# A fused attention, gated-MLP and convolution kernel: one tile of the output projection, parts of the first batch's softmax, and the second MLP's weight prefetch are put at other places in their engines' orders

## The chip, the cores and the metric

One NeuronCore of a Trainium2 chip runs the whole program. The metric is the device time of one execution in microseconds (us), the median over several executions; lower is better. The program has five instruction streams that run side by side and meet only at semaphores: TensorE (PE, matrix products; its weight loads are listed as PEld), VectorE (DVE), ScalarE (ACT), GpSimd (POOL) and SyncE (SP, which here only issues DMAs). ACT issues some DMAs too.

## The reference

```python
# q, k, v: (8, 8, 576, 64); first MLP: w_in 512x1024, w_out 512x512, w_sg 576x576;
# second MLP: w_in2 512x1024, conv_w 3x1024, w_out2 1024x512
q_s = exp(q - max(q, -1)); q_s = q_s / (sum(q_s, -1) + 1e-9)      # softmax over the head's 64
k_s = exp(k - max(k, 2));  k_s = k_s / (sum(k_s, 2) + 1e-9)       # softmax over the sequence
kv = einsum('bhsd,bhse->bhde', k_s, v)
x = einsum('bhsd,bhde->bhse', q_s, kv)           # then heads side by side: (8, 576, 512)
h = gelu_tanh(x @ w_in); u, v = h[..., :512], h[..., 512:]
v_n = (v - mean(v)) / sqrt(var(v) + 1e-6) * g_ln
v_s = einsum('ts,bsd->btd', w_sg, v_n) + b_sg[None, :, None]
x = x + (u * v_s) @ w_out
h = maximum(x @ w_in2, 0)
conv_out = sum over k of conv_w[k] * h shifted by k - 1 along the sequence
out = (h * sigmoid(conv_out)) @ w_out2
```

## The kernel before

The kernel goes through the eight batches of the first MLP (with the attention in front of it) one after another, and then through the eight batches of the second MLP. Each of its float32 matrix products is made of three passes over operands that are split in two parts: a "hi" part that ACT writes by rounding (functions named `hi_...`) and a "lo" part, the difference, that DVE writes (functions `lo_...`). A matrix product of 128x128 by 576 columns is thus three passes of two matmuls with 288 columns each, six matmuls of line L549.

In the first part, `body(m, a, n)` of each engine works on batch m, on the attention of batch a = m + 1, and on the first softmax steps of batch n = m + 2. Batch 0 has a `first_attention()` and its own branches (`start`); batch 7 has `a is None`. Nothing schedules this at run time: every engine's order is the order in which its function is written, and each step waits for semaphores (`e.wait_ge`) that other engines' steps raise. A wait blocks everything behind it on its engine.

The steps that matter here, for batch m and with f from 0 to 3 for four tiles of 128 gated features:

- PE: `sg_unit(m, f)` makes the sequence mixing of tile f (its last matmuls are line L715). Then `o_part(m, d, fs)` adds the products of the gated tiles `fs` to output block d, six matmuls for each f. Before its first tile f it waits for `g_lo` of that tile, `o_part(m, 1, ...)` first waits for `sg_affine` of tile 3 (line L1526) and `o_part(m, 2, ...)` for `kv_lo` (line L1450) of the next batch. After that come `x_piece(a, 0)` and the last output block. In batch 0 the PE also transposes the next batch's q (`turn_q`, L610, which needs `q_norm`, and from the third on `q_lo`) and multiplies exp(k) by v (`kv_piece`, L628, which needs `k_exp`).
- DVE: `affine(m, f)` (L1526) reads the result of `sg_unit`, `lo_g(m, f)` (L1533) writes the lo part of a gated tile and raises `g_lo`, `lo_q_rows(a, d)` (L1430) writes a lo part of the next batch's q, `add_x(m, d)` (L1550 and L1557, for the last block L1542 and L1547) adds the residual and raises `o_add` and `o_last`, and `lo_w2(n)` (L1571) writes a lo part of the second MLP's weights. In batch 0, `sum_q` (L1342, L1345, L1348) makes the reciprocal of a softmax sum, and `lo_w_out` is L1515.
- POOL: `gate(m, f)` (L1882) multiplies the tile by the affine result. In batch 0, `sub_q` (L1821) and `sub_k` (L1839) subtract the maxima of two tiles or the last one, and `scale_q` (L1826) multiplies by the reciprocal.
- ACT: exponentials, hi parts, `gelu`, and `store_x1(m, d)` (L1016), which issues the DMA that stores output block d of the first MLP from one of two buffers `x1`. `add_x(m, 2)` and `add_x(m, 3)` wait for the landing of the stores 0 and 1 of the same batch before they write those buffers again. `hi_w2(n)` (L1021) writes a hi part of the second MLP's weights.
- SP: after the last load for the attention it loads the eight chunks of the second MLP's weights (L518) through three staging buffers, with the first x of the second MLP (`load_x2(0)`, 1152 KB, L505) and the move of batch 7's tail (`move_tail`, L449) between them. Before the first chunk it waits for all `q_lo`, and then for this:

```python
            for x in x1_out:
                e.wait_ge(x, 32 * (B - 2) + 16)
```

With B = 8 this is met when stores 0 and 1 of batch 6 have landed. Chunks 3 and later each wait for `w2_lo`, which `lo_w2` raises.

## Time and profile before

| | us |
|---|---|
| median of 3 executions | 910.94 |
| lowest, highest | 910.55, 912.44 |
| profiled execution, its own time | 912.44 |
| profiled execution, span from first to last instruction | 910.6 |
| PE busy | 894.2 (98%) |
| DVE, ACT, POOL busy | 620.2, 398.4, 368.7 |

The profiled execution is one of the three: its own time is 1.8 us over its span, and 1.5 us over the median. The first MLP with the attention takes the span up to about 503 us, batch 0 up to about 94 us and each of the batches 1 to 6 some 59.4 us; the rest is the second MLP. The page lists work by line and engine; the timeline lists instructions with their start, their duration, and in brackets how long the engine was idle before them and who ended that. Durations in it include time in which an instruction stood still after it had started.

### The profile page before, as it was taken

The numbers are of one execution on the slowest core, as the hardware profiler recorded it, in microseconds if no ns is written. First come the engines' busy times: TensorE is split into PE (matmuls) and PEld (weight loads), VectorE is DVE, ScalarE is ACT, GpSimd is POOL, SyncE is SP. The second block draws the span as 40 slices with busy tenths as digits, with TensorE's granted clock in tenths as the row PEclk, the third lists the DMA queues.
The fourth block names the chain that finished last, engine by engine and source line by source line (L and its number), as shares of the span: only waits on it lengthen the run. The fifth ranks groups of instructions, "written<-read, shape, count | busy, mean of one in ns | idle before, by whom it ended". The sixth has DMA issues, their size and how long they took to land.

```text
span 910.6 us, 15155 instructions
## 1 busy us (share of the span) xinstructions
PE 894.2 (98%) x6132; PEld 831.8 (91%) x6132; DVE 620.2 (68%) x952; ACT 398.4 (44%) x593; POOL 368.7 (40%) x233
## 2 busy tenths in 40 slices
PE   6999999999999999999999999999999999999998
PEld 5798899999999999999999999999999999998986
DVE  6787958578597585875656797866575676757550
ACT  6652553445445445355254354434343343434331
POOL 5764566354572753736232133232232222232220
PEclk9999999999999999999999999999999999999999
DMA  9726674565554735553232202110202020200001
GB/s 298 217 85 203 197 203 147 146 189 171 157 197 127 216 120 154 165 157 83 95 131 70 106 1 87 55 44 12 87 13 87 24 76 24 76 24 24 24 34 47
DMA packets 60037, 99.59 MB, mean 109 GB/s; under 512 B 6720, under 2 KB 25408, under 8 KB 58304
## 3 DMA queue, kind: packets, MB, share of 16 engines
q1 hardware_dynamic: 55360, 89.20, 32.0%
q10 hardware_dynamic: 4608, 9.44, 2.7%
q8 instruction: 48, 0.79, 0.4%
q14 instruction: 21, 0.17, 0.1%
HBM read 78.46 MB, written 19.11 MB: 107 GB/s over the span
## 4 chain that ended last, share of the span: by engine, by line
PE 91%; DVE 3%; POOL 2%; issue 2%; ACT 1%; DMA 1%; SPq 0%; POOLq 0%; DVEq 0%; ACTq 0%
PE psum L549 55%; PE psum L541 30%; PE psum L628 2%; PE psum L715 2%; PE psum L665 1%; POOL plain_arena L1839 1%; DMA plain_arena<-in_q_first 1%; PE psum L587 1%; POOL plain_arena L1882 0%; DVE split_arena L1571 0%; POOL plain_arena L1821 0%; DVE split_arena L1563 0%; DVE plain_arena L1322 0%; POOL plain_arena L1859 0%; DVE plain_arena L1470 0%
## 5 line engine op out<-in xcount | busy, mean ns | idle before, releaser
L549 PE MATMUL psum<-split_arena 128*128 128x288 f32 x4032 | 555.4, 296 | 2.0 <-DVE split_arena L1450 0.9
L549 PEld LDWEIGHTS psum<-split_arena 128*128 128x128 f32 x4032 | 544.6, 189 | 9.0 <-issue 2.0
L541 PE MATMUL psum<-split_arena 128*128 128x512 f32 x1248 | 294.3, 390 | 0.1
L541 PEld LDWEIGHTS psum<-split_arena 128*128 128x128 f32 x1248 | 230.6, 188 | 46.7 <-DVE plain_arena L1547 0.6
L1961 POOL TENSOR_TENSOR plain_arena<-plain_arena 128x576 f32<-128x576 f32 x64 | 107.7, 1683 | 279.2 <-ACT plain_arena L1081 279.2
L1592 DVE SCALAR_TENSOR_TENSOR plain_arena<-plain_arena 128x576 f32<-128x576 f32 x64 | 96.2, 1503 | 2.2
L1587 DVE TENSOR_SCALAR plain_arena<-plain_arena 128x576 f32<-128x576 f32 x64 | 36.0, 563 | 86.6 <-ACT plain_arena L1075 86.6
L1075 ACT ACTIVATE plain_arena<-psum 128x576 f32<-128x576 f32 x64 | 41.6, 650 | 106.6 <-PE psum L549 68.9
L1871 POOL TENSOR_TENSOR plain_arena<-plain_arena 128x2 f32<-128x2 f32 (+1 forms) x24 | 20.4, 850 | 126.6 <-DVE plain_arena L1487 126.6
L1882 POOL TENSOR_TENSOR plain_arena<-plain_arena 128x576 f32<-128x576 f32 x32 | 48.4, 1513 | 52.5 <-DVE plain_arena L1526 52.5
L1081 ACT ACTIVATE plain_arena<-plain_arena 128x576 f32<-128x576 f32 x64 | 43.7, 683 | 42.6 <-DVE split_arena L1765 39.5
L1765 DVE TENSOR_TENSOR split_arena<-plain_arena,split_arena 128x576 fp32r<-128x576 f32 x64 | 53.2, 832 | 10.6 <-ACT split_arena L1087 9.7
L1255 ACT ACTIVATE plain_arena<-psum 128x512 f32<-128x512 f32 x36 | 21.4, 594 | 84.8 <-PE psum L541 84.8
L1589 DVE SCALAR_TENSOR_TENSOR plain_arena<-plain_arena 128x576 f32<-128x576 f32 x64 | 56.0, 875 | 2.3
L1533 DVE TENSOR_TENSOR split_arena<-plain_arena,split_arena 128x576 fp32r<-128x576 f32 x32 | 36.4, 1138 | 21.1 <-ACT split_arena L1012 20.3
L1087 ACT ACTIVATE split_arena<-plain_arena 128x576 fp32r<-128x576 f32 x64 | 43.1, 674 | 8.1 <-POOL plain_arena L1961 8.1
L1839 POOL TENSOR_TENSOR plain_arena<-plain_arena 128x1024 f32<-128x1024 f32 (+1 forms) x21 | 44.2, 2135 | 0.0
L1876 POOL TENSOR_TENSOR split_arena<-plain_arena,split_arena 128x1024 fp32r<-128x1024 f32 (+1 forms) x21 | 41.9, 2020 | 5.1 <-DVE plain_arena L1501 5.1
L1832 POOL TENSOR_TENSOR plain_arena<-plain_arena,split_arena 128x576 f32<-128x576 f32 x24 | 43.1, 1815 | 0.7 <-DMA split_arena<-q_rec_dram 0.5
L1425 DVE TENSOR_TENSOR plain_arena<-plain_arena,split_arena 128x576 f32<-128x576 f32 x24 | 16.6, 753 | 37.2 <-POOL split_arena L1876 37.2
L960 ACT ACTIVATE split_arena<-psum 128x576 fp32r<-128x576 f32 x32 | 20.8, 651 | 47.6 <-PE psum L549 47.4
L1526 DVE SCALAR_TENSOR_TENSOR plain_arena<-psum,plain_arena 128x576 f32<-128x576 f32 x32 | 25.9, 810 | 21.0 <-PE psum L715 21.0
(107 smaller groups left out, 778.7 us busy)
## 6 DMA issues: line engine op xcount, KB each, us to landing
x_dram<-plain_arena ACTq DMA_DIRECT2D x32, 288.0 KB, 2.1
plain_arena<-x_dram SPq DMA_DIRECT2D x8, 1152.0 KB, 5.9
out_rows<-plain_arena SPq DMA_DIRECT2D x36, 256.0 KB, 2.0
plain_arena<-in_kT SPq DMA_DIRECT2D x7, 1152.0 KB, 5.3
plain_arena<-in_k SPq DMA_DIRECT2D x7, 1024.0 KB, 7.1
plain_arena<-in_v SPq DMA_DIRECT2D x28, 256.0 KB, 4.0
plain_arena<-in_q_heads SPq DMA_DIRECT2D x6, 1152.0 KB, 8.4
split_arena<-q_max_dram SPq DMA_DIRECT2D x12, 576.0 KB, 6.3
```

Source lines behind the costliest of these rows:

```text
L541: mm = e.matmul(out, stat[s], mov[m], start=first and n == 0, stop=last and n == 2, skip_group_check=True)
L549: mm = e.matmul(out[:, h, 0:NH], stat[s], mov[m][:, h * NH:(h + 1) * NH], start=first and n == 0, stop=last and n == 2, skip_group_check=True)
L1081: e.activation(gt[:, f % 2, :], cv[:, f % 2, :], ACT.Sigmoid).then_inc(h_gate, 1)
L1087: e.activation(hg(0, par, f), gt[:, f % 2, :], ACT.Identity).then_inc(hg_hi, 1)
L1589: e.scalar_tensor_tensor(out=out, in0=h[:, 0:T], scalar=conv[:, f, 0:1], in1=out, op0=ALU.mult, op1=ALU.add).then_inc(conv_chain, 1)
L1592: e.scalar_tensor_tensor(out=out, in0=h[:, 2:T + 2], scalar=conv[:, f, 2:3], in1=out, op0=ALU.mult, op1=ALU.add).then_inc(h_conv, 1)
L1765: e.tensor_tensor(hg(1, par, f), gt[:, f % 2, :], f32(hg(0, par, f)), ALU.subtract).then_inc(hg_lo, 1)
L1832: e.tensor_tensor(q_rows[:, d, :], q_rows[:, d, :], f32(qT[0][:, d, :]), ALU.mult).then_inc(q_rows_norm, 1)
L1839: e.tensor_tensor(kn[0:rows, t:t + n, :], kn[0:rows, t:t + n, :], kmax_all[0:rows, :].unsqueeze(1).to_broadcast([rows, n, D]), ALU.add).th ...
L1876: e.tensor_tensor(vn[1][0:rows, t:t + n, :], vg[0:rows, t:t + n, :], f32(vn[0][0:rows, t:t + n, :]), ALU.subtract).then_inc(vn_lo, 1)
L1882: e.tensor_tensor(uT[:, f, :], uT[:, f, :], tmp[:, f % 2, :], ALU.mult).then_inc(gate_done, 1)
L1961: e.tensor_tensor(gt[:, f % 2, :], gt[:, f % 2, :], hp[:, f % 2, 1:T + 1], ALU.mult).then_inc(hg_full, 1)
```

## The change

Seven orders are changed; no instruction is added, removed or resized. One wait is removed.

- SP: the wait for the `x1` stores before the weight chunks is gone, and chunk 5 is issued before the move of batch 7's tail and not behind it.
- PE, in every batch: output block 2 takes its tiles 0, 1 and 2 in one piece behind tile 2 of the blocks 0 and 1.
- DVE, batches 1 to 6: `lo_q_rows(a, 1)` stands ahead of `lo_g(m, 2)`.
- DVE, POOL and ACT in batch 0: the second `sub_q`, `exp_q` and `sum_q` come earlier, the second `sub_k` and `exp_k` later, and the first `lo_g` ahead of the first two `lo_q`.
- ACT and DVE in batch 7: `hi_w2(0..2)` and `lo_w2(0..2)` are all at its head, the first two `hi_w2` ahead of `hi_x(7, 2)`.

```diff
             e.wait_ge(q_lo, q_lows(B))
-            for x in x1_out:
-                e.wait_ge(x, 32 * (B - 2) + 16)
             for n, (src, hi, lo) in enumerate(W2):
                 if n == 3:
                     load_x2(0)
-                if n == 5:
+                if n == 6:
                     move_tail(B - 1)
...
-                for fs in ([0, 1], [2], [3]):
-                    for d in range(DT - 1):
+                for fs in ([0, 1], [2]):
+                    for d in range(2):
                         o_part(m, d, fs)
+                o_part(m, 2, [0, 1, 2])
+                for d in range(DT - 1):
+                    o_part(m, d, [FT - 1])
...
+                if a is None:
+                    hi_w2(0)
+                    hi_w2(1)
                 if not start:
                     hi_x(m, DT - 2)
                 if a is None:
-                    hi_w2(0)
-                    hi_w2(1)
+                    hi_w2(2)
...
                     e.wait_ge(u_done, B * FT)
-                    hi_w2(2)
                     hi_w2(3)
                     hi_w2(4)
                 if start:
                     exp_q(a, 0)
                     exp_k(a, 0)
-                    exp_k(a, 1)
-                    tile(0)
                     exp_q(a, 1)
-                    tile(1)
...
                     if start:
                         if f == 1:
+                            tile(0)
+                            tile(1)
+                            exp_k(a, 1)
                             exp_q(a, 2)
...
                 elif a is None:
-                    for w in range(2):
+                    for w in range(3):
                         lo_w2(w)
...
                     sum_q(a, 0)
                     affine(m, 0)
+                    sum_q(a, 1)
                     affine(m, 1)
+                    lo_g(m, 0)
                     tile(0)
-                    sum_q(a, 1)
                     tile(1)
-                    lo_g(m, 0)
...
                     if a is None:
-                        lo_w2(2)
                         lo_w2(3)
...
                     affine(m, 3)
+                    if a is not None:
+                        lo_q_rows(a, 1)
                     lo_g(m, 2)
                     if a is not None:
-                        lo_q_rows(a, 1)
                         lo_q_rows(a, 2)
...
                     sub_q(a, 0)
                     sub_k(a, 0)
-                    sub_k(a, 1)
+                    sub_q(a, 1)
                     scale_q(a, 0)
-                    sub_q(a, 1)
...
                     if start and f == 0:
                         scale_q(a, 1)
+                        sub_k(a, 1)
                         sub_q(a, 2)
```

PE, the output projection of batch 1 (the other batches are alike), with the waits. Before (L549 is the helper that records every such matmul):

```order
L549 MATMUL psum<-split_arena 128x288 [waits g_lo,sg_affine]
L549 MATMUL psum<-split_arena 128x288 x5
L549 MATMUL psum<-split_arena 128x288 [waits g_lo]
L549 MATMUL psum<-split_arena 128x288 x5
L549 MATMUL psum<-split_arena 128x288 [waits sg_affine]
L549 MATMUL psum<-split_arena 128x288 x11
L549 MATMUL psum<-split_arena 128x288 [waits kv_lo,v_gelu]
L549 MATMUL psum<-split_arena 128x288 x11
L549 MATMUL psum<-split_arena 128x288 [waits g_lo]
L549 MATMUL psum<-split_arena 128x288 x17
L549 MATMUL psum<-split_arena 128x288 [waits g_lo]
```

The same place of the changed kernel, whose lines are numbered two lower here (L547):

```order
L547 MATMUL psum<-split_arena 128x288 [waits g_lo,sg_affine]
L547 MATMUL psum<-split_arena 128x288 x5
L547 MATMUL psum<-split_arena 128x288 [waits g_lo]
L547 MATMUL psum<-split_arena 128x288 x5
L547 MATMUL psum<-split_arena 128x288 [waits sg_affine]
L547 MATMUL psum<-split_arena 128x288 x11
L547 MATMUL psum<-split_arena 128x288 [waits g_lo]
L547 MATMUL psum<-split_arena 128x288 x11
L547 MATMUL psum<-split_arena 128x288 [waits kv_lo,v_gelu]
L547 MATMUL psum<-split_arena 128x288 x17
L547 MATMUL psum<-split_arena 128x288 [waits g_lo]
```

The third wait for `g_lo` (tile 2) now stands behind 24 matmuls and not behind 36, the wait for `kv_lo` behind 36 and not 24, and the wait for tile 3 behind 54 as before.

DVE, the end of batch 1's gated tiles (batches 2 to 6 are alike). Before, `affine` 2, `lo_kv`, `affine` 3, `lo_g` 2, two `lo_q_rows`, `lo_g` 3:

```order
L1526 SCALAR_TENSOR_TENSOR plain_arena<-psum,plain_arena 128x576
L1450 TENSOR_TENSOR split_arena<-psum,split_arena 64x4x64 x2
L1526 SCALAR_TENSOR_TENSOR plain_arena<-psum,plain_arena 128x576
L1533 TENSOR_TENSOR split_arena<-plain_arena,split_arena 128x576
L1430 TENSOR_TENSOR split_arena<-plain_arena,split_arena 128x576 x2
L1533 TENSOR_TENSOR split_arena<-plain_arena,split_arena 128x576
```

The same place of the changed kernel, numbered two higher here (`lo_g` is L1535, `lo_q_rows` L1432):

```order
L1528 SCALAR_TENSOR_TENSOR plain_arena<-psum,plain_arena 128x576
L1452 TENSOR_TENSOR split_arena<-psum,split_arena 64x4x64 x2
L1528 SCALAR_TENSOR_TENSOR plain_arena<-psum,plain_arena 128x576
L1432 TENSOR_TENSOR split_arena<-plain_arena,split_arena 128x576
L1535 TENSOR_TENSOR split_arena<-plain_arena,split_arena 128x576
L1432 TENSOR_TENSOR split_arena<-plain_arena,split_arena 128x576
L1535 TENSOR_TENSOR split_arena<-plain_arena,split_arena 128x576
```

`lo_g` of tile 2 is now the second step behind the last `affine`, and the first is `lo_q_rows`, of the same shape.

POOL, the softmax of batch 1 during batch 0. Before (`sub_q`, twice `sub_k`, `scale_q`, `sub_q`, `gate`, `scale_q`, `sub_q`):

```order
L1821 TENSOR_TENSOR plain_arena<-plain_arena 128x1024
L1839 TENSOR_TENSOR plain_arena<-plain_arena 128x1024 x2
L1826 TENSOR_TENSOR plain_arena<-plain_arena 128x1024
L1821 TENSOR_TENSOR plain_arena<-plain_arena 128x1024
L1882 TENSOR_TENSOR plain_arena<-plain_arena 128x576
L1826 TENSOR_TENSOR plain_arena<-plain_arena 128x1024
L1821 TENSOR_TENSOR plain_arena<-plain_arena 64x512
```

The same place of the changed kernel, numbered two higher:

```order
L1823 TENSOR_TENSOR plain_arena<-plain_arena 128x1024
L1841 TENSOR_TENSOR plain_arena<-plain_arena 128x1024
L1823 TENSOR_TENSOR plain_arena<-plain_arena 128x1024
L1828 TENSOR_TENSOR plain_arena<-plain_arena 128x1024
L1884 TENSOR_TENSOR plain_arena<-plain_arena 128x576
L1828 TENSOR_TENSOR plain_arena<-plain_arena 128x1024
L1841 TENSOR_TENSOR plain_arena<-plain_arena 128x1024
L1823 TENSOR_TENSOR plain_arena<-plain_arena 64x512
```

The second `sub_k` has moved from the third place to the seventh, behind the second `scale_q`.

## Rows read from the trace of the kernel before

**Rows 1.** The page, busy time and share of the span by engine.
```profile
PE 894.2 (98%) x6132; PEld 831.8 (91%) x6132; DVE 620.2 (68%) x952; ACT 398.4 (44%) x593; POOL 368.7 (40%) x233
```
**Rows 2.** The waits of PE: total us, times, longest us.
```profile
PE psum L610 <- POOL plain_arena L1826: 1.8, 2, 1.3
...
PE psum L549 <- DVE split_arena L1450: 0.9, 1, 0.9
...
PE psum L549 <- DVE plain_arena L1526: 0.3, 1, 0.3
```
**Rows 3.** The chain of waits: start, us, what; batches 2 and 3.
```profile
198.28 14.40 PE psum L549 x108
...
245.26 3.20 PE psum L549 x24
...
257.71 14.40 PE psum L549 x108
```
**Rows 4.** Timeline of PE, output projection of batch 0: start, us, what.
```profile
77.04 1.84 PE L549 MATMUL psum<-split_arena 128*128 128x288 f32 x12
79.20 1.85 PE L549 MATMUL psum<-split_arena 128*128 128x288 f32 x12 [0.31 <-DVE plain_arena L1526]
81.94 0.37 PE L549 MATMUL psum<-split_arena 128*128 128x288 f32 x1 [0.89 <-DVE split_arena L1450]
```
**Rows 5.** Timelines of DVE and then POOL in batch 0.
```profile
54.95 3.42 DVE L1515 TENSOR_TENSOR split_arena<-plain_arena,split_arena 128x1024 fp32r<-128x1024 f32 x1
...
59.53 1.13 DVE L1345 TENSOR_SCALAR plain_arena<-plain_arena 128x16 f32<-128x16 f32 x1
...
57.23 3.38 POOL L1839 TENSOR_TENSOR plain_arena<-plain_arena 128x1024 f32<-128x1024 f32 x1
...
61.02 1.90 POOL L1826 TENSOR_TENSOR plain_arena<-plain_arena 128x1024 f32<-128x1024 f32 x1 [0.40 <-DVE plain_arena L1348]
...
67.71 1.90 POOL L1826 TENSOR_TENSOR plain_arena<-plain_arena 128x1024 f32<-128x1024 f32 x1 [1.53 <-DVE plain_arena L1348]
```
**Rows 6.** Timelines of PE, DVE and POOL where batch 6's output projection begins.
```profile
435.87 14.56 PE L549 MATMUL psum<-split_arena 128*128 128x288 f32 x108
...
436.81 0.75 DVE L1533 TENSOR_TENSOR split_arena<-plain_arena,split_arena 128x576 fp32r<-128x576 f32 x1
436.97 1.88 POOL L1882 TENSOR_TENSOR plain_arena<-plain_arena 128x576 f32<-128x576 f32 x1 [1.14 <-DVE plain_arena L1526]
...
437.47 2.00 DVE L1430 TENSOR_TENSOR split_arena<-plain_arena,split_arena 128x576 fp32r<-128x576 f32 x1
```
**Rows 7.** Timelines of PE and DVE at one short wait for `g_lo`, batch 7.
```profile
499.22 1.33 PE L549 MATMUL psum<-split_arena 128*128 128x288 f32 x6
...
499.08 0.75 DVE L1533 TENSOR_TENSOR split_arena<-plain_arena,split_arena 128x576 fp32r<-128x576 f32 x1
```
**Rows 8.** Landing of the L1016 stores, windows 440:460 and 498:512; timeline around them.
```profile
DMA to landing us min/median/max: 2.1/3.4/6.2
...
DMA to landing us min/median/max: 2.1/3.5/4.0
...
449.43 1.66 SPq L518 DMA_DIRECT2D plain_arena<-in_w_in  x3
...
506.69 0.76 DVE L1557 TENSOR_TENSOR plain_arena<-psum,split_arena 128x576 f32<-128x576 f32 x1 [1.88 <-DMA x_dram<-plain_arena]
```
**Rows 9.** Timeline from batch 6 into batch 7.
```profile
440.73 0.74 DVE L1430 TENSOR_TENSOR split_arena<-plain_arena,split_arena 128x576 fp32r<-128x576 f32 x1
...
445.73 0.33 ACTq L1016 DMA_DIRECT2D x_dram<-plain_arena  x1
...
448.69 0.76 DVE L1557 TENSOR_TENSOR plain_arena<-psum,split_arena 128x576 f32<-128x576 f32 x1
...
450.18 0.46 DVE L1547 TENSOR_TENSOR plain_arena<-psum,split_arena 128x288 f32<-128x288 f32 x1
450.27 2.90 PE L541 MATMUL psum<-split_arena 128*128 128x512 f32 x12
```

## The prediction, made before the changed kernel ran

> **What bounds the kernel now.** I read the page's busy times first: TensorE is busy for 894.2 of 910.6 us [rows 1]. No other engine is a bound, so an edit is worth what it takes from, or adds to, PE's waits. The list of PE's waits comes next: behind the first loads, which the change leaves alone, only three kinds are left that an edit touches, `turn_q` waiting for POOL's `scale_q` (1.8 us in two waits), and in the output projection one wait for `lo_kv` and one for `affine` [rows 2]. All of these lie in batch 0. The chain of waits shows the rest: batches 2 and 3 begin their output projection at 198.28 and 257.71, 59.43 us apart, and both have the same unbroken 14.40 us of 108 matmuls, 0.133 us each; 24 of them take 3.20 us [rows 3]. Where PE never waits there is nothing to gain, and every wait that the change brings in is paid in full, once per batch. So I looked at each moved step for two things: does PE stop waiting in batch 0, and does it begin to wait in batches 1 to 7.
>
> **Batch 0, output projection: 1.7 us less.** Twelve matmuls need 1.60 us by [rows 3]. The first twelve start at 77.04 and the next ones at 79.20, 2.16 us later: 0.56 us lost for `affine` of tile 3. The next start at 81.94 instead of 80.80: 1.14 us lost for `kv_lo` [rows 4]. The second wait goes for certain: with the new order `kv_lo` is needed twelve matmuls (1.6 us) later, and the tile 2 that is needed in its place is ready before the third affine, since it stands ahead of it on DVE. The first wait goes only if `affine` 3 comes 0.6 us earlier. It stands behind the whole chain of softmax steps and gates, and I follow that chain now.
>
> **Batch 0, softmax steps: about 0.1 us less for PE.** What rules here is how DVE and POOL stop each other. DVE's L1515 takes 3.42 us while POOL's L1839 runs before it, L1839 then takes 3.38 us, and the small L1345 takes 1.13 us although it has 16 elements a partition and ends at 60.66, when POOL's instruction ends at 60.61 [rows 5]. So of two such instructions one stands still until the other is finished, and the one that waits goes next. With this reading I put the new order through. The second `sub_q` starts at 57.23, stands until L1515 ends at 58.37 and runs 1.9 us (taken from L1826, the same shape and kind of operands) to 60.2. L1345 ends then, not at 60.66, so the first `scale_q` starts at 60.6 instead of 61.02 and `turn_q` 0 is 0.4 us earlier. The second `sum_q` follows 3 us earlier than before, and the second `scale_q` ends at about 66.2 instead of 69.61, which takes away the other of `turn_q`'s waits (0.5 to 0.7 us). But the second `sub_k` now stands behind it: 66.2, plus 0.6 us for a `lo_g` that waits for the same release, plus some 2.3 us of its own (3.38 less the 1.14 that it stood still), is 69.1; `exp_k` adds 1.1, and `kv_piece` 2 can start at 70.2. Before it started at about 70.3. A wait for `sub_k` takes the place of the wait for `scale_q`: 0.1 us gained, from 0.1 lost to 0.6 gained if `sub_k` is not held up. The rest of the chain (`gate` 1 and 2, `lo_g` 2) then comes 0.9 to 1.1 us earlier, and `affine` 3 ends at about 78.1, in time for 78.6. I take the full 1.7 us, so batch 0 gives **-1.8 us**, between -1.1 (`affine` 3 as late as now) and -2.3. The loads of batch 2 that follow have landed when their steps start, as far as I can shift them.
>
> **Batches 1 to 6: a new wait, 3.4 us more.** PE needs tile 2 of `g_lo` after 24 matmuls instead of 36. At the same time `lo_q_rows` 1 goes in front of it. In batch 6 the projection starts at 435.87, so the tile is due at 435.87 + 3.20 = 439.07. Today DVE makes it at 436.81 to 437.56, ahead of POOL's last `gate`, which starts at 436.97 and stands still until DVE is done (1.88 us); the next DVE instruction, `lo_q_rows`, starts at 437.47 and then stands behind the gate, 2.00 us, to 439.47 [rows 6]. Both DVE instructions are 128x576 with two SBUF inputs, and their inputs have long been there. Swapped, the first takes 0.75 us, the gate is served, and the second, now `lo_g` 2, ends at 439.47: 0.40 us after it is due. What such a wait costs beyond that is shown in batch 7: `lo_g` ends at 499.83, the fourth of six matmuls that start at 499.22 is due at 499.62, 0.21 us earlier, and the six take 1.33 us instead of 0.96 (six starts of 0.133 and 0.16 for the last one's end), 0.37 lost [rows 7]. So add 0.16 for the restart: 0.56 us in each of the batches 2 to 6 (the same order, and their rows differ by 0.1 us at most), and about 0.6 in batch 1. Six times 0.57 is **+3.4 us**. The bounds: nothing, if `lo_g` 2 gets in ahead of the gate (it would then end at 438.3), and 4.2 if the gate takes a little more. I take 3.4, since the row is the same pair of instructions at the same moment. The steady part has no wait further on that could absorb this.
>
> **Into batch 7: the weight loads meet the stores, 0.8 us more.** The wait that is removed held the first chunks back to 449.43 [rows 8]. The remaining wait, `q_lo`, ends with `lo_q_rows` 3 at 441.47 [rows 9], so three chunks and x (2688 KB together) are issued from 441.5 on, 7.9 us earlier, and are on their way when batch 6's stores 0 and 1 are issued at 445.73 (446.3 with that batch's new wait) and 1.5 us later. Alone such a store lands in 2.1 us, beside the loads in up to 6.2; beside the x load in the end of batch 7 in 4.0, and there DVE stood for 1.88 us in `add_x` [rows 8]. With 4.7 us for the first and 4.2 for the second (between these) they land at 451.0 and 452.0. `add_x` 2 then writes at 451.0 and not at 449.25 (448.69 + 0.56 [rows 9]), ends at 451.8, and `add_x` 3 raises `o_last` at 452.7 instead of 451.2 (450.64 + 0.56). PE wants it after six matmuls of the twelve that start at 450.27 (0.23 us each), so at 452.2 with the shift. That makes 0.5 us, and 0.3 for the restart and for the second half of `add_x`: **+0.8 us**. If both stores land in 3.5 us there is no wait at all; if they need 6.2, `o_last` comes at 454.5 and PE loses 2.3. The loads themselves gain nothing: PE does not wait for a weight today. `hi_w2` 0 and 1 ahead of `hi_x(7, 2)` take 2.1 us of ACT (1.05 each) that ACT has free before x is ready, the third `lo_w2` ends 0.2 us before `moments` starts: both at zero, and up to 0.5 us if the x chain is pushed by the late stores.
>
> The Trainium skill speaks against this term. "DMA: Bandwidth & Descriptors", section "Queues, rings and completion order", says that each DMA engine takes turns between the queues that it has work for, packet by packet. The stores go through another queue than the loads; by that rule they would get half of the engines at least, and land near the lower row, not the upper. The 6.2 us of this trace speaks against it, the 3.5 and 4.0 for it.
>
> **Sum.** -1.8 + 3.4 + 0.8 = +2.4 us. The profiled execution would go from 912.44 to 914.8. Its time stands 1.5 us over the median, so for the median I take 910.94 + 2.4 = **913.3 us**. I call 0.2% (1.8 us) the least that a measurement of this kernel can tell from no change: slower begins at 912.8, faster at 909.1.
>
> **Rivals.** (1) The stores share fairly: they land 3.5 us after issue, `o_last` is in time, and the third term is zero: 910.9 - 1.8 + 3.4 = 912.5, within 0.2%. The stores of 3.5 and 4.0 us beside a load speak for it, the 6.2 against it. (2) No new wait in the steady batches: POOL's gate and DVE meet in another way than in [rows 6], `lo_g` 2 is ready at 438.3, and the change keeps its gain: 910.9 - 1.8 + 0.8 = 909.9, or 909.1 and faster if (1) holds too. Against it stand six batches with the same pattern; for it, that a release of 0.4 us decides. (3) The late stores push the whole x chain: `o_last` at 454.5 and later, 2.3 us and more: 914.8. It decides from landings of over 5.5 us. (4) `affine` 3 doesn't come earlier, and 0.56 us of batch 0 stays: 913.9.
>
> **How the numbers follow.** The forecast has 0.45, (1) 0.27, (2) 0.12, (3) 0.09, (4) 0.07. Faster needs (2) together with (1): 0.06. The forecast, (3) and (4) lie over 912.8, but the forecast is near the bound, so that of its 0.45 I leave 0.08 to the middle: slower 0.53. The rest, 0.41, is within 0.2%. The range goes from 911.5 (the steady wait half as long in (1)) to 915.0 (over (3)).
>
> **What would show it.** In PE's waits: L549 behind DVE's `lo_g` (L1535), six times about 0.4 us, and `lo_g` of tile 2 with 2.0 us in the timeline where it had 0.75. PE's wait behind L1450 gone, and that behind `affine` gone; `turn_q`'s two waits replaced by one smaller and a wait of L628 for the `exp_k` behind `sub_k`. The chain's batch period goes from 59.43 to 60.0. The stores of batch 6 take over 3.5 us, with an idle time of DVE before `add_x`. The prediction is wrong if the period stays at 59.4, or if PE stands for more than 2 us between 450 and 458.

## The result, and the profile of the changed kernel

The changed kernel takes 915.91 us (median of 6 runs, 915.07 to 918.02), the kernel before 911.05 us on the same chip (6 runs, 910.55 to 912.44). The ratio is 1.0053, with a 95% interval of 1.0040 to 1.0066: **slower by 0.53%, or 4.9 us**, twice the forecast change and above its range. The profiled execution has a span of 914.4 us and its own time is 916.24 us, 3.8 us over that of the kernel before (910.6 and 912.44). Line numbers of the changed kernel differ by two to three from those before: L547 is the old L549, L539 the old L541, L1535 (`lo_g`) the old L1533, L1432 (`lo_q_rows`) the old L1430, L1559 and L1549 (both halves of `add_x`) the old L1557 and L1547.

The page, busy time by engine; TensorE is busy for 1.0 us more than in [rows 1], while the span grew by 3.8:

```profile
PE 895.2 (98%) x6132; PEld 831.3 (91%) x6132; DVE 619.3 (68%) x952; ACT 398.7 (44%) x593; POOL 368.7 (40%) x233
```

The waits of PE (total us, times, longest us), to be laid beside [rows 2]:

```profile
PE psum L547 <- DVE split_arena L1535: 2.3, 6, 0.9
PE psum L539 <- DVE plain_arena L1549: 1.4, 1, 1.4
PE psum L608 <- POOL plain_arena L1828: 0.8, 1, 0.8
PE psum L626 <- ACT plain_arena L930: 0.8, 1, 0.8
PE psum L547 <- DVE split_arena L1458: 0.5, 1, 0.5
```

The two waits of the output projection in batch 0 are gone. The `turn_q` waits have shrunk from 1.8 to 0.8, and one of 0.8 for ACT's `exp_k` has come. Two kinds are new: PE waits six times for `lo_g`, and once, for 1.4 us, for `add_x`.

To put a place on every microsecond, I took the start of the same matmul in both traces (the 540th, the 644th and so on; a program gives the same order of matmuls on PE in all kernels here, apart from the order of tiles inside one projection) and how far it had moved. The difference from one place to the next, changed kernel less kernel before, in us:

| stretch | difference |
|---|---|
| start-up, which the change leaves alone | +0.1 |
| batch 0, softmax steps | -0.2 |
| batch 0, output projection | -1.7 |
| batch 1, before its projection | +0.4 |
| batch 1, output projection | +1.1 |
| batches 2 to 6, output projections (five times 0.54) | +2.7 |
| from batch 6 into batch 7, about 450 to 462 | +1.9 |
| first steps of the second MLP, about 514 to 546 | -0.5 |
| sum | +3.8 |

Both profiled executions had a slow start-up: in eleven of the twelve runs below, which leave it alone too, it is 0.3 to 1.8 us shorter. That fits the profile of before, which stands 1.4 us over its median. That of the changed kernel stands only 0.3 over its own, so that elsewhere it was probably a cheap one; the second profile of it, below, shows a place.

In batch 1, the four other profiles with the same pair of edits have 0.5 us and not 1.1. The trace shows where the rest comes from: POOL stood for 2.17 us for the load of `q_rec_dram`, which landed at 129.5 (0.48 us and 127.9 in the second profile of the same kernel, `e13_after_again`), the gate of tile 2 started 1.1 us later, and `lo_g` of tile 2, which waits for it through ACT, ended at 141.41 and not at 140.96. This is read from two traces; no run tested it.

**Batch 0.** The timeline of PE, the stretch of [rows 4]: start, us, what.

```profile
70.18 0.69 PE L626 MATMUL psum<-plain_arena 128*64 128x65 f32 x16 [0.79 <-ACT plain_arena L930]
...
76.92 9.33 PE L547 MATMUL psum<-split_arena 128*128 128x288 f32 x68
```

`kv_piece` 2 starts at 70.18, behind a wait for `exp_k`, and the projection then runs without a gap. POOL and DVE, in two timelines, show the order worked out for [rows 5]:

```profile
66.13 2.91 POOL L1841 TENSOR_TENSOR plain_arena<-plain_arena 128x1024 f32<-128x1024 f32 x1
...
77.25 0.81 DVE L1528 SCALAR_TENSOR_TENSOR plain_arena<-psum,plain_arena 128x576 f32<-128x576 f32 x1
```

The second `sub_k` ends at 69.04 (forecast 69.1), and `affine` 3 at 78.06 (forecast 78.1).

**The steady batches.** Timelines of PE, DVE and POOL in batch 6, which answer to [rows 6]:

```profile
437.72 3.36 PE L547 MATMUL psum<-split_arena 128*128 128x288 f32 x24
441.37 5.85 PE L547 MATMUL psum<-split_arena 128*128 128x288 f32 x42 [0.29 <-DVE split_arena L1535]
...
438.66 0.75 DVE L1432 TENSOR_TENSOR split_arena<-plain_arena,split_arena 128x576 fp32r<-128x576 f32 x1
439.32 2.00 DVE L1535 TENSOR_TENSOR split_arena<-plain_arena,split_arena 128x576 fp32r<-128x576 f32 x1
...
438.82 1.88 POOL L1884 TENSOR_TENSOR plain_arena<-plain_arena 128x576 f32<-128x576 f32 x1 [1.14 <-DVE plain_arena L1528]
```

The 2.00 us behind POOL's gate, which `lo_q_rows` bore before, is now on `lo_g` of tile 2. It ends at 441.32; the 24 matmuls that need no tile 2 took until 440.92 (437.72 and 3.20), and the next starts at 441.37. The chain of waits goes through these steps in each of the batches 2 to 6 now (two of them shown), and answers to [rows 3]:

```profile
199.49 1.93 DVE split_arena L1535
...
201.46 11.45 PE psum L547 x84
...
259.47 1.92 DVE split_arena L1535
...
261.44 8.65 PE psum L547 x63
```

201.46 to 261.44 is 59.98 us a batch, where it was 59.43.

**From batch 6 into batch 7.** The timeline of the queues, DVE and PE at the place of [rows 8] and [rows 9] (SPq and ACTq are the stretches in which the queue's engine issued the DMAs; L516 are the three weight chunks, L505 is x, L1017 are the stores of batch 6's x1):

```profile
443.35 1.29 SPq L516 DMA_DIRECT2D plain_arena<-in_w_in  x3
...
444.75 0.38 SPq L505 DMA_DIRECT2D plain_arena<-x_dram  x1
...
448.12 0.33 ACTq L1017 DMA_DIRECT2D x_dram<-plain_arena  x1
...
449.65 5.41 ACTq L1017 DMA_DIRECT2D x_dram<-plain_arena  x2
...
452.66 1.54 PE L539 MATMUL psum<-split_arena 128*128 128x512 f32 x6
...
453.95 0.76 DVE L1559 TENSOR_TENSOR plain_arena<-psum,split_arena 128x576 f32<-128x576 f32 x1 [2.98 <-DMA x_dram<-plain_arena]
...
455.12 0.46 DVE L1549 TENSOR_TENSOR plain_arena<-psum,split_arena 128x288 f32<-128x288 f32 x1
...
455.63 1.83 PE L539 MATMUL psum<-split_arena 128*128 128x512 f32 x6 [1.42 <-DVE plain_arena L1549]
```

Store 0 is issued at 448.12 and DVE's `add_x` 2, which may overwrite its buffer only when it has landed, starts at 453.95: 5.8 us. DVE stood for 2.98 us, `add_x` 3 came late, and PE stopped in the middle of its twelve matmuls. Landing of the L1017 stores, window 440:460, where [rows 8] had 6.2 at most, but for a store of which nobody had to wait:

```profile
DMA to landing us min/median/max: 2.1/3.6/5.8
```

### The profile page after: what moved, and what is told of

The parts are those of the page before. It is cut to its first block, busy times and chain, and to the rows that moved or that the text cites. A ratio compares the mean times of both kernels' runs of the same rounds, so it can differ in the third digit from the quotient of the medians.

```text
span 914.4 us, 15154 instructions
## 1 busy us (share of the span) xinstructions
PE 895.2 (98%) x6132; PEld 831.3 (91%) x6132; DVE 619.3 (68%) x952; ACT 398.7 (44%) x593; POOL 368.7 (40%) x233
## 4 chain that ended last, share of the span: by engine, by line
PE 84%; DVE 7%; POOL 3%; issue 2%; DMA 2%; ACT 1%; SPq 0%; POOLq 0%; DVEq 0%
PE psum L547 50%; PE psum L539 29%; PE psum L626 2%; PE psum L713 1%; DVE split_arena L1535 1%; PE psum L663 1%; POOL plain_arena L1841 1%; DMA split_arena<-q_rec_dram 1%; DMA x_dram<-plain_arena 1%; DMA plain_arena<-in_q_first 1%; PE psum L585 1%; DVE plain_arena L1472 1%; POOL plain_arena L1823 1%; POOL plain_arena L1884 1%; POOL split_arena L1878 0%
## 5 line engine op out<-in xcount | busy, mean ns | idle before, releaser
L547 PE MATMUL psum<-split_arena 128*128 128x288 f32 x4032 | 556.7, 296 | 3.0 <-DVE split_arena L1535 2.3
L547 PEld LDWEIGHTS psum<-split_arena 128*128 128x128 f32 x4032 | 545.0, 189 | 11.0 <-DVE split_arena L1535 4.0
L539 PE MATMUL psum<-split_arena 128*128 128x512 f32 x1248 | 294.9, 391 | 1.6 <-DVE plain_arena L1549 1.4
L539 PEld LDWEIGHTS psum<-split_arena 128*128 128x128 f32 x1248 | 230.5, 188 | 48.8 <-DVE plain_arena L1549 2.8
L1767 DVE TENSOR_TENSOR split_arena<-plain_arena,split_arena 128x576 fp32r<-128x576 f32 x64 | 53.2, 832 | 10.7 <-ACT split_arena L1088 9.7
L1535 DVE TENSOR_TENSOR split_arena<-plain_arena,split_arena 128x576 fp32r<-128x576 f32 x32 | 40.7, 1272 | 23.0 <-ACT split_arena L1013 22.2
L1088 ACT ACTIVATE split_arena<-plain_arena 128x576 fp32r<-128x576 f32 x64 | 43.1, 674 | 8.1 <-POOL plain_arena L1963 8.1
L1013 ACT ACTIVATE split_arena<-plain_arena 128x576 fp32r<-128x576 f32 x32 | 21.9, 686 | 42.5 <-POOL plain_arena L1884 42.3
```

The source lines that it names most:

```text
L539: mm = e.matmul(out, stat[s], mov[m], start=first and n == 0, stop=last and n == 2, skip_group_check=True)
L547: mm = e.matmul(out[:, h, 0:NH], stat[s], mov[m][:, h * NH:(h + 1) * NH], start=first and n == 0, stop=last and n == 2, skip_group_check=True)
L1088: e.activation(hg(0, par, f), gt[:, f % 2, :], ACT.Identity).then_inc(hg_hi, 1)
L1535: e.tensor_tensor(gT[1][:, f, :], uT[:, f, :], f32(gT[0][:, f, :]), ALU.subtract).then_inc(g_lo, 1)
L1767: e.tensor_tensor(hg(1, par, f), gt[:, f % 2, :], f32(hg(0, par, f)), ALU.subtract).then_inc(hg_lo, 1)
```

## Experiments

Differences by stretch are those of the table above: to the kernel before, by the start of the same matmul, in us. Medians are given with that of the kernel before on the same chip.

### The steady wait: two edits apart and together

`e1_tile_order` is the kernel before with the new order of the tiles on PE alone:

```diff
-                for fs in ([0, 1], [2], [3]):
-                    for d in range(DT - 1):
+                for fs in ([0, 1], [2]):
+                    for d in range(2):
                         o_part(m, d, fs)
+                o_part(m, 2, [0, 1, 2])
+                for d in range(DT - 1):
+                    o_part(m, d, [FT - 1])
```

> The kernel before, with the new order of output tiles on PE alone (block 2 takes tiles 0 to 2 behind the others). Theory: the wait for kv_lo in batch 0 goes (1.14 us), the wait for affine there stays (0.56), and the steady batches keep their period of 59.43 us, because lo_g of tile 2 still ends at 437.56 on the scale of batch 6, 1.5 us before PE wants it: about 1.1 us less than before, 909.9. Rival (the earlier need of tile 2 is by itself too early): the period goes to about 60.0 as in the changed kernel, 3 us more, 913 or so.

`e2_swap` is the kernel before with the swap on DVE alone:

```diff
-                    lo_g(m, 2)
                     if a is not None:
                         lo_q_rows(a, 1)
+                    lo_g(m, 2)
+                    if a is not None:
                         lo_q_rows(a, 2)
```

> The kernel before, with lo_q_rows 1 ahead of lo_g 2 on DVE in batches 1 to 6 alone. Theory: lo_g 2 takes 2.0 us instead of 0.75 behind the gate, but PE wants it only behind 36 matmuls, 1.2 us after it is there: no wait, the same time as before within 0.3 us, period 59.43. Rival (the late lo_g 2 by itself makes PE wait): 0.5 us more in each of six batches, 3 us in all.

`e3_both` has these two edits and no other:

> The kernel before, with the new order of output tiles and the swap on DVE together, and nothing else. Theory: one new wait of PE for L1533 in each of the batches 1 to 6, 0.54 us each, some 3.3 us, less the 1.14 of kv_lo: about 2.2 us more than before. If the batch 1 wait is 1.1 us as in the changed kernel, it is of the pair itself and the sum is 2.7; if it is 0.6, the longer wait there came from the loads that the change of batch 0 moved. Rival (the two don't work together): the sum of the two runs before this one.

| | median, before | ratio (interval) | batch 0 projection | batch 1 projection | batches 2 to 6, each |
|---|---|---|---|---|---|
| tile order | 911.21, 912.21 | 0.9993 (0.9983 to 1.0004) | -1.11 | 0 | 0 |
| swap | 911.82, 912.21 | 1.0002 (0.9994 to 1.0011) | -0.02 | 0 | 0 |
| both | 914.16, 912.21 | 1.0030 (1.0019 to 1.0042) | -1.13 | +0.53 | +0.54 |

The waits of PE for `lo_g` in the kernel with both; neither of the other two has such a row:

```profile
PE psum L549 <- DVE split_arena L1536: 1.7, 6, 0.3
```

With the swap alone, the timeline of DVE shows the late `lo_g` (L1533) too, at no cost:

```profile
436.89 1.99 DVE L1533 TENSOR_TENSOR split_arena<-plain_arena,split_arena 128x576 fp32r<-128x576 f32 x1
```

It ends at 438.88, and PE wants the tile after 36 matmuls there, 1.6 us later than with the new order of tiles. Each edit alone is free. The pair costs 0.54 us a batch: the one makes the tile due 1.6 us earlier, the other makes it ready some 1.9 us later. The tile order alone also brings the 1.1 us of `lo_kv` in batch 0, as forecast, and leaves the wait for `affine` (0.3 in PE's waits).

### The loads that no longer wait for the stores

`e4_no_store_wait` is the kernel before with one edit on SP:

```diff
             e.wait_ge(q_lo, q_lows(B))
-            for x in x1_out:
-                e.wait_ge(x, 32 * (B - 2) + 16)
```

> The kernel before, with the wait for the x1 stores in front of the weight loads taken away, and nothing else. Theory: the loads start some 7.9 us earlier (441.5), the stores of output blocks 0 and 1 of batch 6 take 5 to 6 us instead of 2.1, and PE stands 2 to 2.5 us (more than the 1.9 of the changed kernel, where PE's own wait of 0.5 us covers a part) for add_x (L1547) at about 451. Rival (the queues share fairly, the stores land in about 3.5 us): no wait of PE over 0.3 us, the same time as before.

916.50 us against 912.21, ratio 1.0061 (1.0048 to 1.0073). In the profile, this one edit costs 5.6 us between 449 and 462 (0.6 of it comes back later in batch 7 and 0.3 at the start of the second MLP). Timeline of the queues, DVE and PE:

```profile
442.03 0.38 SPq L505 DMA_DIRECT2D plain_arena<-x_dram  x1
...
444.86 0.33 ACTq L1014 DMA_DIRECT2D x_dram<-plain_arena  x1
...
446.39 7.58 ACTq L1014 DMA_DIRECT2D x_dram<-plain_arena  x2
...
449.40 1.54 PE L539 MATMUL psum<-split_arena 128*128 128x512 f32 x6
...
452.86 0.76 DVE L1555 TENSOR_TENSOR plain_arena<-psum,split_arena 128x576 f32<-128x576 f32 x1 [5.14 <-DMA x_dram<-plain_arena]
...
454.54 2.00 PE L539 MATMUL psum<-split_arena 128*128 128x512 f32 x6 [3.59 <-DVE plain_arena L1545]
```

The stores of 288 KB took 8.0 us (444.86 to 452.84) and 7.1 us (446.39 to 453.50), and the first packet of store 0 moved at 449.17, 4.3 us after its issue. Six matmuls after 449.40 PE was due at 450.8 and went on at 454.54: 3.7 us lost. The other 1.9 us come after the wait. The granted clock is the share of TensorE's full clock that the profile records. The windows of this kernel (stretch, us, busy time and count of PE, PEld, DVE, ACT, POOL, then the granted clock, the DMA share and GB/s):

```profile
453.00:455.00 2.00, 0.46 (x2) 0.42 (x3) 1.93 (x5) 0.65 (x1) 0.00 (x0) 1.00 0.26 99
455.00:457.00 2.00, 2.00 (x9) 1.48 (x8) 1.01 (x2) 0.00 (x0) 0.00 (x0) 0.76 0.51 195
457.00:459.00 2.00, 2.00 (x8) 1.78 (x7) 0.30 (x1) 0.98 (x2) 0.00 (x0) 0.50 0.01 1
459.00:463.00 4.00, 4.00 (x20) 3.38 (x19) 0.46 (x1) 2.22 (x3) 0.00 (x0) 0.94 0.00 0
```

After the wait the granted clock falls to 0.50 (1.2 instead of 2.4 GHz) and stays there for 3.4 us in all (0.96 us of the second stretch, the whole third, 0.48 of the fourth). Six matmuls of 288 columns take 1.65 us in it where they take 0.95 at full clock.

`e13_after_again` is the changed kernel once more, on another chip, to see how much this place varies:

> The changed kernel once more, for a second profile. Theory: the six waits for L1535 are the same to 0.05 us each in batches 2 to 6, and what differs between executions are the waits that hang on landings: at 450 to 458 between 1 and 4 us, in batch 1 between 0.2 and 1.5 us, and a stretch at the lower clock (0.5) wherever PE stood for 3 us or more. Rival: all waits are the same, and the difference between executions lies in the first 40 us alone.

917.12 us against 912.01, ratio 1.0049 (1.0032 to 1.0065). Its runs go from 912.85 to 918.98; this profiled execution has a span of 917.1 us. Waits of PE first, then the windows of the same place, and the ACT queue:

```profile
PE psum L539 <- DVE plain_arena L1549: 3.7, 2, 3.0
PE psum L547 <- DVE split_arena L1535: 1.7, 6, 0.3
```

```profile
454.00:457.00 3.00, 0.26 (x1) 0.26 (x2) 1.68 (x4) 0.65 (x1) 0.00 (x0) 1.00 0.28 105
457.00:459.00 2.00, 2.00 (x8) 1.37 (x8) 1.18 (x3) 1.04 (x2) 0.00 (x0) 0.76 0.30 114
459.00:461.00 2.00, 2.00 (x9) 1.81 (x9) 0.00 (x0) 1.59 (x4) 0.00 (x0) 0.50 0.09 33
```

```profile
449.18 5.71 ACTq L1017 DMA_DIRECT2D x_dram<-plain_arena  x2
```

The same program, and the steady wait is the same as in `e3_both` to a hundredth. But the stores took 6.1 and 6.9 us, and the stretch cost 5.1 us and not 1.9, with the lower clock in it. Of the two waits for L1549 only the one of 3.0 us is here; from due time to restart PE lost 3.2 us, and the other 1.9 come behind it, as in `e4_no_store_wait`. The first profile of the changed kernel had the wait of 1.42 us here, and its clock stayed at 1.00. So this term is not one number: it was 1.9 us in one execution and 5.1 in another, which fits medians that differ by more (4.9 us) than the first pair of profiles (3.8). The mean granted clock of the eight executions says the same: 1.000 in the fastest, 912.85 us, 0.998 or 0.996 in the other seven (3.4 us at 0.50 take 0.002 from the mean). In that fastest one the term may well have been under 1.9 us; it has no trace.

The other wait for L1549, of 0.7 us, is in batch 0, where `add_x` 3 waits for a store that was issued beside the load of v:

```profile
93.30 1.83 PE L539 MATMUL psum<-split_arena 128*128 128x512 f32 x6 [0.72 <-DVE plain_arena L1549]
```

It is the same kind of race. Three more profiles have this wait (0.5 us in `e8_x_late`, 0.9 in `e7_back_wait`, 0.4 in `e12_x_in_four`), and the last of them leaves batch 0 as it was.

### What in front of the store holds it: x, or the DMA's size

In `e8_x_late`, the changed kernel, the wait for the stores stands between the three chunks and x:

```diff
             for n, (src, hi, lo) in enumerate(W2):
                 if n == 3:
+                    for x in x1_out:
+                        e.wait_ge(x, 32 * (B - 2) + 16)
                     load_x2(0)
```

> The changed kernel, with the wait for the x1 stores put between the first three weight chunks and the load of x, so that the chunks (1536 KB) stay early and the 1152 KB of x are issued behind the stores. Theory (the stores stand behind whatever is queued, of which x is the part still on its way when they are issued): chunks are through at about 449 and the stores of blocks 0 and 1 land in 2.1 to 3.5 us, PE's wait for o_last at 454 is under 0.3 us instead of 1.6, 1.6 us less than the changed kernel. Rival (it is the chunks that hold the stores up): the stores still take over 4.5 us and PE stands as in the changed kernel.

In `e14_x_alone_early`, the kernel before, x alone goes ahead of the wait (1152 KB early, the chunks late):

```diff
+            load_x2(0)
             for x in x1_out:
                 e.wait_ge(x, 32 * (B - 2) + 16)
             for n, (src, hi, lo) in enumerate(W2):
-                if n == 3:
-                    load_x2(0)
```

> The kernel before, with the load of x alone issued early (as soon as q_lo allows, 441.5), and the weight chunks behind the wait for the x1 stores as before. Theory (the bytes still queued when the stores are issued count): x is through at about 447, 2 us after the first store is issued, so the first store takes 3 to 4 us and the second 2 to 3, and PE stands under 0.5 us. Rival (a load of x beside a store is bad whatever its rest): the first store takes over 5 us, PE stands over 1 us.

And `e12_x_in_four` is `e4_no_store_wait` with x in four DMAs of 288 KB (ACT's wait for x is raised to match the four):

```diff
+                if b == 0:
+                    for d in range(DT):
+                        e.dma_start(x2_raw(b)[:, d, :], x1_dram[b, d * P:(d + 1) * P, :]).then_inc(x2_in, 16)
+                    return
```

> The kernel before, without the wait for the x1 stores (as e4_no_store_wait), with the load of x in four DMAs of 288 KB instead of one of 1152 KB, issued one behind the other. Theory (what is queued in bytes ahead of the stores holds them up): the stores take 7 to 8 us and PE stands 3 to 4 us, as in e4_no_store_wait. Rival (the one long DMA holds them up, not its bytes): the stores take under 5 us, PE stands under 1.5 us.

| | loads queued before store 0 | stores 0 and 1 | 450 to 462 | median, before, ratio (interval) |
|---|---|---|---|---|
| `e8_x_late` | 1536 KB, 4.8 us before | 2.3, 2.1 us | 0 | 913.21, 911.67, 1.0021 (1.0012 to 1.0031) |
| `e14_x_alone_early` | 1152 KB, 4.2 us before | 2.1, 3.4 us | 0 | 911.95, 912.01, 0.9998 (0.9988 to 1.0008) |
| `e4_no_store_wait` | 2688 KB, 4.2 us before | 8.0, 7.1 us | +5.64 | 916.50, 912.21, 1.0061 (1.0048 to 1.0073) |
| `e12_x_in_four` | 2688 KB, 4.2 us before | 6.9, 7.3 us | +6.30 | 914.57, 912.01, 1.0025 (1.0012 to 1.0038) |

The "before" of the second column is from the first load's issue to the store's. A reader sees the difference in one row of the ACT queue, that of stores 1 and 2, where the second can be issued only when `add_x` 2 has run. `e8_x_late`, then `e14_x_alone_early`, then `e12_x_in_four`:

```profile
447.74 2.56 ACTq L1019 DMA_DIRECT2D x_dram<-plain_arena  x2
```

```profile
446.79 2.54 ACTq L1015 DMA_DIRECT2D x_dram<-plain_arena  x2
```

```profile
447.01 6.54 ACTq L1018 DMA_DIRECT2D x_dram<-plain_arena  x2
```

Either part of the loads alone costs nothing here, and both together hold the store until they are nearly through: in `e4_no_store_wait` x landed at 453.03 and store 0 at 452.84. What differs is how much is still to be moved for SP when the store is issued. By the packets of the traces, 0.2 and 0.3 MB of the loads had not started then in `e14_x_alone_early` and `e8_x_late`, and 1.4 to 1.7 MB in `e4_no_store_wait`, `e12_x_in_four` and both profiles of the changed kernel. And in all seven traces in which loads were issued ahead of store 0, it landed close to the last of them: from 0.2 us before it (`e4_no_store_wait`) to 0.9 us behind it (`e14_x_alone_early`), in the changed kernel 0.4 us behind it (453.93 and 453.53). That is a reading of seven traces, not a rule of the queues; what decides the order between them was not measured apart.

One long DMA is not needed for this: in the profiled execution of `e12_x_in_four` four short ones held the store as long. But that execution, 918.09 us, was the slowest of its six (median 914.57), and its ratio of 1.0025 lies clear of the 1.0061 of `e4_no_store_wait`. So in most executions the four short DMAs cost less than the one long one, and why was not tested.

### Is it the wait alone? The loads and `hi_w2` belong together

`e7_back_wait` is the changed kernel with only that wait restored. I expected the third term to go:

> The changed kernel with the wait for the x1 stores put back, all else as changed. Theory: the 1.9 us between 450 and 458 go, the six waits for L1535 stay (3.8 us): about 1.9 us less than the changed kernel, 1.9 to 2.0 us more than before. Rival (the late landing only hides another wait behind it, hi_w2 ahead of hi_x): 1 us or more of PE's wait stays there.

915.41 us against 911.67, ratio 1.0042 (1.0029 to 1.0055). The term only shrank, from +1.9 (or +5.1) to +1.4. The timeline of ACT and DVE:

```profile
456.50 1.06 ACT L1024 ACTIVATE split_arena<-plain_arena 128x1024 fp32r<-128x1024 f32 x1 [2.88 <-DMA plain_arena<-in_w_in]
457.93 1.06 ACT L1024 ACTIVATE split_arena<-plain_arena 128x1024 fp32r<-128x1024 f32 x1 [0.37 <-DMA plain_arena<-in_w_in]
458.89 0.63 ACT L963 ACTIVATE split_arena<-psum 128x576 fp32r<-128x576 f32 x1
459.56 0.76 DVE L1460 TENSOR_TENSOR split_arena<-psum,split_arena 128x576 fp32r<-128x576 f32 x1 [4.91 <-ACT split_arena L963]
```

`hi_w2` 0 and 1 (L1024 in this kernel) now stand ahead of `hi_x(7, 2)` (L963) on ACT and wait for chunks that the restored wait makes late. They hold the x chain, and PE waits for DVE's L1460. Early loads need the wait gone, and the moved `hi_w2` needs early loads: these two parts of the change can only be judged together. No run undoes the `hi_w2` move by itself; that it is the cause here is read from these rows.

`e6_back_both` also undoes the swap, so that neither the steady wait nor, as I thought, the stores should cost:

> The changed kernel with two of its edits undone: lo_g 2 stands ahead of lo_q_rows 1 again, and the wait for the x1 stores stands before the weight loads again. Theory: no wait of PE for L1535 except where batch 1's gate is late (0.1 us or less), no wait at 450 to 455, batch 0's gain of 1.8 us less 0.4 in batch 1 stays: 1.4 us less than before or a little more, period 59.43. Rival (the change loses something else that neither undone edit explains): the same time as before, or more.

911.36 us against 911.67, ratio 1.0004 (0.9993 to 1.0015). The steady wait is gone, as expected (0 in batches 2 to 6). At 450 to 462 it still lost 1.64 us, and the cause is the one just shown, `PE psum L549 <- DVE split_arena L1460` with 1.9 us in PE's waits.

### The softmax order alone, and a version that keeps the gains

`e9_softmax_order` is the kernel before with the moves of the softmax steps in batch 0 only (all edits with `sub_k`, `scale_q`, `sum_q`, `exp_k`, `tile`, and `lo_g(m, 0)` in the start branch):

> The kernel before, with the new order of batch 0's softmax steps on DVE, ACT and POOL alone. Theory: turn_q starts 0.4 us earlier, kv_piece 2 then waits for exp_k, affine 3 comes 0.9 us earlier and its wait (0.56) goes, and the wait for kv_lo stays, shorter: kv_lo itself comes about 1.1 us earlier and PE 0.7 us earlier, so 0.4 of 1.14 go: about 1.1 us less at the end of batch 0's projection. In batch 1 the x chain then gives 0.3 to 0.4 back. Its gate 1 comes late if the load of q in 77 to 86 us is what moved; with that order alone DVE is not swapped, so PE has no wait there.

910.63 us against 911.67, ratio 0.9989 (0.9980 to 0.9998). It gives -0.21 in the softmax steps and -1.12 in the projection: the wait for `affine` is gone, and that for `lo_kv` fell from 0.9 to 0.4. The tile order (-1.11) and this (-1.12) overlap, since together they give -1.66 to -1.68.

`e10_x_late_back_swap` is `e8_x_late` with the swap on DVE undone:

> The changed kernel with lo_g 2 ahead of lo_q_rows 1 again, and the load of x (but not the weight chunks) held until the stores of blocks 0 and 1 have landed. Theory: all of the change's losses are gone (the six waits, the wait at 450 to 458), its gains in batch 0 stay: 1.8 us less there, 0.2 to 1 us given back in batch 1, 0.5 us less at 500, so 1.3 to 2.0 us less than before, and 4 to 5 us less than the changed kernel. Rival (a loss is left that the ledger by segments doesn't show): the same time as before or more.

910.44 us against 912.01, ratio 0.9981 (0.9971 to 0.9991), a span of 907.3: faster than the kernel before by 0.19%, at the edge of what can be told, and faster than the changed kernel by about 0.7%. By stretch: -0.23 and -1.68 in batch 0, 0 in the batches 2 to 6, 0 at 450 to 462, and -0.6 at 470 to 500, which `e8_x_late` and `e4_no_store_wait` have too and nothing here explains (of the span another 1.8 us are the start-up alone). It gives back 0.84 us in batch 1, where PE waits for ACT:

```profile
PE psum L549 <- ACT plain_arena L988: 0.7, 1, 0.7
```

## Why the prediction was wrong, point by point

- **What bounds the kernel, and the sign: right.** PE is the bound, each wait that came in was paid in full and, in the steady part, once per batch. The kernel became slower.
- **Batch 0, -1.8 us: right** (-0.2 and -1.7, sum -1.9; -1.9 in the five other profiles with the same edits). The order worked out hit `sub_k`, `kv_piece` 2 and `affine` 3 to 0.1 us. The reading of [rows 5], that of two such instructions one stands still and the waiting one goes next, carried this.
- **Behind batch 0, taken at nothing: not quite.** "The loads of batch 2 that follow have landed when their steps start, as far as I can shift them": with batch 0 about 2 us earlier, the stretch before batch 1's projection lost 0.2 to 1.1 us in the six profiles that have the whole new order of batch 0 (0.4 in the first profile), 0.3 with the tile order alone and 0.0 with the softmax order alone. But `e12_x_in_four`, which leaves batch 0 alone, lost 0.5 there, so part of this is chance and not the change. In four profiles (`e13_after_again`, `e8_x_late`, `e7_back_wait`, `e12_x_in_four`) the wait there is the one for a store beside a load shown above; in `e10_x_late_back_swap` it is for ACT, and what sets it was not tested.
- **Batches 1 to 6, +3.4 us: right in kind and nearly in size.** Six times 0.57 was forecast, and 0.54 came in each of batches 2 to 6 and, in four other profiles, 0.53 to 0.54 in batch 1. The first profile of the changed kernel has 1.11 in batch 1, where a load landed 1.6 us later than in the second and `lo_g` ended later.
- **The stores, +0.8 us: here the prediction failed.** The mechanism is the one described, down to `add_x` 2 held and `add_x` 3 raising `o_last` late, and rival (3), with 0.09, was the case that came ("It decides from landings of over 5.5 us": 5.8, 6.1 and, with the one edit alone, 8.0). The size was wrong by two steps. The first is "With 4.7 us for the first and 4.2 for the second (between these)". The row of 6.2 us was not a far bound but the nearest case: it is the store issued at 451.54, with all 2688 KB issued ahead of it from 449.43 on. The 4.7 us row is the store issued at 449.48, just behind the first chunk, and the 4.0 us row had x alone beside it. Two rows of before at that place, behind that of the three chunks in [rows 8], and the store's size and landing by the row of its issue:

```profile
451.19 0.68 SPq L505 DMA_DIRECT2D plain_arena<-x_dram  x1
...
451.54 0.33 ACTq L1016 DMA_DIRECT2D x_dram<-plain_arena  x1
...
x_dram<-plain_arena ACTq DMA_DIRECT2D x1, 288.0 KB, 6.2
```

  With 6.2 us the prediction's own working has PE losing 2.3 us, and in the first profile the stretch cost 1.9. Even 6.2 was no upper bound: the stores took up to 8.0. Second, the cost of a PE stop was counted as its length and 0.3 for the restart and `add_x`. That holds for the first profile (1.6 from due time to restart, and 0.3). In `e4_no_store_wait` and `e13_after_again` PE stood for 3.6 and 3.0 us and then ran at half clock for 3.4 us, which costs 1.9 us on top in both. So the term was 1.9 us in one profile of the changed kernel and 5.1 in the other.
- **Rival (1), the fair share.** The forecast leaned on it in part, and rival (1) had 0.27. In these traces store 0 did not get a share from its issue on: its first packet moved 4.3 us after it in `e4_no_store_wait` and 4.0 us in the changed kernel, when all but 0.3 and 0.1 MB of the 2.7 MB of loads had started. The rule that I weighed, from the Trainium skill, "DMA: Bandwidth & Descriptors", section "Queues, rings and completion order" (each DMA engine takes turns between its queues, packet by packet), would have given about 3.5 us; the measurement, 5.8 to 8.0, decides against reading it that way here.
- **`hi_w2` at nothing: right for the change as it is,** but only because the loads are early. `e7_back_wait` shows 1.4 us when they are not.
- **Rivals (2) and (4)** did not come: `lo_g` never got in ahead of the gate, and `affine` 3 came in time.
- **The sum.** +0.1, -1.9, +0.4, +3.8, +1.9 and -0.5 make +3.8 in the first profile. In the second the same terms are -0.3, -1.9, +0.9, +3.2, +5.1 and -0.5, +6.5 in all, as by the span (917.1 us). The medians, +4.9, lie between. The two sums are 1.4 and 4.1 us over the forecast of 2.4; the stores' term is 1.1 and 4.3 us over its forecast of 0.8, so nearly all of the miss is there.

## What to carry to other kernels

Where the bound engine never waits, judge a moved instruction by two times, when it is ready and when it is due, and move only one of the two: here each edit alone was free, and the pair cost 0.54 us in every batch. Before a wait is taken from in front of a load, look at what short transfer another queue has to issue soon after, who stands behind its landing, and how many bytes will still be queued at that moment. Then look for the row whose queue is the most like it and take that, not a value midway between unlike rows: here the like row had 6.2 us, the forecast took 4.7, and 5.8 to 8.0 came. And a long stop of TensorE may cost more than its length: after those of 3.0 and 3.6 us here the granted clock fell, and the sum had no term for it.

## What the runs showed of the hardware

- A store of 288 KB on ACT's queue landed in 2.1 us alone. As store 0 or 1 of batch 6 it landed in 2.1 to 3.4 us with 1152 or 1536 KB issued over 4 us earlier on SP's queue, and in 5.1 to 8.0 us with 2688 KB. With the 2688 KB issued only in the 2.1 us before it, in the kernel before, it was 6.2 us. In one profiled execution four DMAs of 288 KB held it as well as one of 1152 KB.
- Store 0 landed between 0.2 us before and 0.9 us behind the last load issued ahead of it on the other queue, in all seven traces that have one.
- The granted clock was 0.50 for 3.4 us after PE had stood for 3.0 us (`e13_after_again`) and for 3.6 us (`e4_no_store_wait`), and stayed at 1.00 after 1.4 us. In `e12_x_in_four` it was 0.50 for 6.8 us, from the last microsecond of a stop of 3.3 us on. It also was 0.50 for 3.4 us in the start-up of 4 of the 14 traces, both profiles of the changed kernel among them, where PE waits for 5.4 us and then for some 1 us at a time in all of them: the same program does not always pay it.
- One and the same program spread from 912.85 to 918.98 us in eight runs, where the kernel before lies between 910.39 and 914.51 in 29 on the same chip. The term that differs most between the two profiles is the race between two queues, with the clock behind it: such a term should be given as a range.
